# The first matmul of two expert layers on 2x2 blocks with seven products in place of eight

## The chip, the core and the metric

The kernel runs on one core of a Trainium2 chip. Its engines work side by side and meet at semaphores: TensorE (PE; its weight loads have rows of their own, PEld), VectorE (DVE), ScalarE (ACT), GpSimd (POOL) and SyncE (SP), which issues the transfers. The metric is the device time in microseconds (us), the median of several runs; lower is better.

## The reference

```python
qn = q / (np.linalg.norm(q, axis=1, keepdims=True) + 1e-06)      # q, k, v: (1, 6016, 256)
kn = k / (np.linalg.norm(k, axis=1, keepdims=True) + 1e-06)
s = kn.transpose(0, 2, 1) @ qn / tau                             # 256 x 256
a = softmax(s);  x = v @ a                                       # 6016 tokens of 256
h = x @ w_in;  g = h * np.clip(h + 3.0, 0.0, 6.0) / 6.0;  y1 = g @ w_out      # 256 -> 2048 -> 256
h = np.maximum(y1 @ w_in2, 0.0);  y = h * h @ w_out2                          # 256 -> 2048 -> 256
```

## The kernel before

**Opening.** q and k stream in. ACT squares them (L562), DVE adds the squares into `sq_sum`, an SBUF tile of 1024 columns (L689), and PE makes the 256x256 scores (L416). Three of the fourteen loads (`split_loads`) are split into a high and a low float32r half, the low one by POOL (L350, printed as `w_fold_lo`, whose memory it shares). Two short matmuls (L394, L396) sum the squares over partitions, ahead of the last 16 score matmuls. Softmax follows. The attention matrix `a` is folded into `w_in` (`fold`, 8 units of 6 matmuls into `fold_acc`, L442), so that v goes straight into layer 1 ("A"); layer 2 is "B".

**Main part.** Every float32 product is three float32r matmuls: high x high, high x low, low x high. Tokens go in blocks of 512 (eleven, and a last one of 384), printed in PSUM as `hid` (hidden values, 128 x tokens) and `y_acc` (the output). For each block and layer there are 16 chunks `f` of 128 hidden columns. `hidden` is 6 matmuls (L453, L455, L457, twice), since the contraction over 256 is two halves. `contract` is 6 more (L467, L469, L473, twice). In between, ACT makes `ramp` (L626), DVE multiplies it with `hid` (L784 in layer 1, L781 in layer 2), ACT makes the high half `gated_hi` (L631), DVE the low half `gated_lo` (L789). `contract` of chunk f stands behind `hidden` of chunk f+2 (`LAG` = 2). The order on each engine is written out by hand; blocks of layer A and layer B alternate inside a loop (`Fori`). SP loads v per block and stores the output per block; y1 stays on the core. PE waits for `gated_ready` of two chunks ago ahead of `hidden`, and for `gated_hi_ready` and `gated_lo_ready` in `contract`.

## Time and profile before

| | |
|---|---|
| median of 3 runs | 1109.98 us (1108.57 to 1110.26) |
| span of the profiled execution | 1107.8 us, 2.2 us under the median |
| PE busy, share of the span | 1089.1 us, 98%, 4912 matmuls |
| DVE | 648.5 us, 59% |
| ACT | 579.2 us, 52% |
| POOL | 55.2 us, 5% |

The profile has one execution's own span and no separate time for it; the 2.2 us are the distance to the median of the runs. A matmul's row is longer than the distance to the next one, since matmuls are pipelined: what one costs is read from start to start. A full PE says that PE is never without work, not that it runs at its peak.

### The profile page before, as it was taken

How to read it: one execution, taken by the hardware profiler on the slowest of the kernel's cores; microseconds unless marked ns; L12 is line 12 of the kernel's file. 1: busy time of each engine (PE TensorE's matmuls, PEld its weight loads, DVE VectorE, ACT ScalarE, POOL GpSimd, SP SyncE). 2: the span in 40 equal slices, each digit the busy share in tenths (PEclk: the TensorE clock that was granted, in tenths of full speed). 3: DMA queues.
4: the chain of work that ended last, by engine and by line, in shares of the span. 5: the costliest groups of instructions: out<-in, count | busy, mean ns of one | idle time of the engine just before them, and what ended most of it. 6: DMA issues, size and time to landing. Idle time of an engine off the chain costs nothing.

```text
span 1107.8 us, 13572 instructions
## 1 busy us (share of the span) xinstructions
PE 1089.1 (98%) x4912; PEld 914.0 (83%) x4912; DVE 648.5 (59%) x937; ACT 579.2 (52%) x878; POOL 55.2 (5%) x29
## 2 busy tenths in 40 slices
PE   8799999999999999999999999999999999999997
PEld 7678888888888888888888888888888888889887
DVE  5956656555555555655555655655655555556554
ACT  5565565454554554554554554545545455455543
POOL 2360330000000000000000000000000000000000
PEclk9899999999999999999999999999999999999999
DMA  9805000000000000000000000000000000000000
GB/s 353 264 20 170 1 1 20 9 12 15 4 19 0 19 19 0 19 19 0 19 19 0 19 19 0 19 19 0 19 10 9 14 1 19 1 1 20 1 14 20
DMA packets 59351, 33.33 MB, mean 30 GB/s; under 512 B 50369, under 2 KB 54977, under 8 KB 59073
## 3 DMA queue, kind: packets, MB, share of 16 engines
q1 hardware_dynamic: 59328, 33.04, 10.5%
q8 instruction: 14, 0.23, 0.1%
q14 instruction: 9, 0.07, 0.0%
HBM read 26.87 MB, written 6.16 MB: 30 GB/s over the span
## 4 chain that ended last, share of the span: by engine, by line
PE 94%; DVE 3%; ACT 1%; DMA 1%; issue 0%; SPq 0%; DVEq 0%; ACTq 0%
PE hid L453 15%; PE y_acc L473 15%; PE hid L455 15%; PE y_acc L469 15%; PE y_acc L467 15%; PE hid L457 15%; DVE sq_sum L689 3%; PE fold_acc L442 1%; DMA qk<-k_dram 1%; ACT sq L562 0%; PE y_acc L416 0%; ACT w_fold_hi L559 0%; SPq L297 0%; SPq L298 0%; PE y_acc L394 0%
## 5 line engine op out<-in xcount | busy, mean ns | idle before, releaser
L789 DVE TENSOR_TENSOR gated_lo<-gated,gated_hi 128x512 fp32r<-128x512 f32 (+1 forms) x384 | 266.3, 693 | 268.6 <-ACT gated_hi L631 268.6
L631 ACT ACTIVATE gated_hi<-gated 128x512 fp32r<-128x512 f32 (+1 forms) x384 | 239.3, 623 | 292.0 <-DVE gated L781 147.1
L473 PE MATMUL y_acc<-gated_lo,w_out_hi 128*128 128x512 f32 (+1 forms) x768 | 295.4, 385 | 0.0
L469 PE MATMUL y_acc<-gated_hi,w_out_hi 128*128 128x512 f32 (+1 forms) x768 | 295.3, 385 | 0.0
L467 PE MATMUL y_acc<-gated_hi,w_out_lo 128*128 128x512 f32 (+1 forms) x768 | 295.2, 384 | 0.0
L626 ACT ACTIVATE ramp<-hid,zero 128x512 f32<-128x512 f32 (+1 forms) x192 | 130.8, 681 | 103.7 <-PE hid L457 101.4
L784 DVE SCALAR_TENSOR_TENSOR gated<-ramp,hid 128x512 f32<-128x512 f32 (+1 forms) x192 | 129.9, 676 | 87.6 <-ACT ramp L626 86.4
L626 ACT ACTIVATE ramp<-hid,half 128x512 f32<-128x512 f32 (+1 forms) x192 | 130.4, 679 | 97.0 <-PE hid L457 94.6
L781 DVE TENSOR_TENSOR gated<-ramp,hid 128x512 f32<-128x512 f32 (+1 forms) x192 | 130.0, 677 | 76.8 <-ACT ramp L626 75.6
L473 PEld LDWEIGHTS y_acc<-gated_lo,w_out_hi 128*128 128x128 f32 x768 | 144.1, 188 | 27.8 <-DVE gated_lo L789 0.3
L467 PEld LDWEIGHTS y_acc<-gated_hi,w_out_lo 128*128 128x128 f32 x768 | 144.2, 188 | 27.5
L469 PEld LDWEIGHTS y_acc<-gated_hi,w_out_hi 128*128 128x128 f32 x768 | 144.2, 188 | 27.3
L453 PE MATMUL hid<-v_hi,w_fold_hi 128*128 128x512 f32 (+1 forms) x384 | 147.7, 385 | 0.0
L455 PE MATMUL hid<-v_lo,w_fold_hi 128*128 128x512 f32 (+1 forms) x384 | 147.6, 384 | 0.0
L457 PE MATMUL hid<-v_hi,w_fold_lo 128*128 128x512 f32 (+1 forms) x384 | 147.6, 384 | 0.0
L457 PE MATMUL hid<-y_hi,w_in_lo 128*128 128x512 f32 x352 | 137.0, 389 | 0.0
L455 PE MATMUL hid<-y_lo,w_in_hi 128*128 128x512 f32 x352 | 137.0, 389 | 0.0
L453 PE MATMUL hid<-y_hi,w_in_hi 128*128 128x512 f32 x352 | 136.9, 389 | 0.0
L453 PEld LDWEIGHTS hid<-v_hi,w_fold_hi 128*128 128x128 f32 x384 | 72.0, 188 | 14.4 <-issue 0.5
L457 PEld LDWEIGHTS hid<-v_hi,w_fold_lo 128*128 128x128 f32 x384 | 72.1, 188 | 13.8
L455 PEld LDWEIGHTS hid<-v_lo,w_fold_hi 128*128 128x128 f32 x384 | 72.1, 188 | 13.7
L457 PEld LDWEIGHTS hid<-y_hi,w_in_lo 128*128 128x128 f32 x352 | 66.1, 188 | 13.8
(83 smaller groups left out, 607.0 us busy)
## 6 DMA issues: line engine op xcount, KB each, us to landing
v_raw<-v_dram SPq DMA_DIRECT2D x44, 128.0 KB, 2.9
out_dram<-out_sb SPq DMA_DIRECT2D x44, 128.0 KB, 2.5
qk<-q_dram SPq DMA_DIRECT2D x10, 512.0 KB, 11.4
qk<-k_dram SPq DMA_DIRECT2D x10, 512.0 KB, 12.7
raw_a<-w_in_dram SPq DMA_DIRECT2D x4, 512.0 KB, 5.9
raw_b<-w_out_dram SPq DMA_DIRECT2D x1, 2048.0 KB, 12.6
raw_b<-w_in_dram SPq DMA_DIRECT2D x1, 2048.0 KB, 7.7
raw_a<-w_out_dram SPq DMA_DIRECT2D x1, 2048.0 KB, 8.6
```

The source lines that it names most:

```text
L453: nc.tensor.matmul(hid[:, f % 2, 0:n], w_hi[:, m, cols], x_hi[:, m, 0:n], start=(m == 0), stop=False)
L455: nc.tensor.matmul(hid[:, f % 2, 0:n], w_hi[:, m, cols], x_lo[:, m, 0:n], start=False, stop=False)
L457: mm = nc.tensor.matmul(hid[:, f % 2, 0:n], w_lo[:, m, cols], x_hi[:, m, 0:n], start=False, stop=(m == KC - 1))
L467: nc.tensor.matmul(acc[:, m, 0:n], w_lo[:, f, cols], gated_hi[:, r, 0:n], start=(f == 0), stop=False)
L469: nc.tensor.matmul(acc[:, m, 0:n], w_hi[:, f, cols], gated_hi[:, r, 0:n], start=False, stop=False)
L473: mm = nc.tensor.matmul(acc[:, m, 0:n], w_hi[:, f, cols], gated_lo[:, r, 0:n], start=False, stop=(f == NF - 1))
L626: nc.scalar.activation(ramp[:, f % 2, 0:n], hid[:, f % 2, 0:n], ACT.Relu, bias=bias[:, 0:1], scale=scale).then_inc(ramp_ready, 1)
L631: nc.scalar.activation(gated_hi[:, f % GATE_RING, 0:n], gated[:, f % 2, 0:n], ACT.Copy) \
L689: nc.vector.tensor_tensor(sq_sum[:, :, 0:n, :], sq_sum[:, :, 0:n, :], sq[:, s % SQ_RING, :, 0:n, :], ALU.add).then_inc(summed, 1)
L781: nc.vector.tensor_tensor(gated[:, f % 2, 0:n], ramp[:, f % 2, 0:n], hid[:, f % 2, 0:n], ALU.mult).then_inc(gated_ready, 1)
L784: nc.vector.scalar_tensor_tensor(out=gated[:, f % 2, 0:n], in0=ramp[:, f % 2, 0:n], scalar=1.0, in1=hid[:, f % 2, 0:n], op0=ALU.min, op1=A ...
L789: nc.vector.tensor_tensor(gated_lo[:, f % GATE_RING, 0:n], gated[:, f % 2, 0:n], gated_hi[:, f % GATE_RING, 0:n].bitcast(F32), ALU.subtrac ...
```

## The change

**Blocks.** Tokens now go in pairs of blocks (six pairs: five of 2 x 512, the last of 2 x 448), and the 2048 hidden columns in eight groups of 256. For one pair and one group, the hidden values are four tiles of 128 x tokens: C11, C12, C21, C22. They were eight block products (of 3 matmuls each); they are now seven products of sums of blocks. The weights need four sums and differences per block (T/S combinations, seven operands in all, `wi_hi` and `wi_lo`), and so does x (`combine_x`, four subtractions, and seven high and seven low halves per pair, `xs_hi` and `xs_lo`).

**Sums of products.** The tiles are put together in PSUM. `seed` (ACT) copies the first product from `bank_a` to `bank_b`, where the third accumulates on it. `keep_p5` (ACT) takes the second out to `p5_sb`. `seed_u4` (DVE) adds `bank_b` and `p5_sb` into `bank_c`; `add_22` (DVE) adds them into `h22` in SBUF once more has accumulated. `bank_b` and `bank_c` print as `bank_bc`, `p5_sb` as `p_sb`, `h22` as `h_61`.

**Order.** One layer at a time over all tokens: six steps of eight groups for layer 1, six for layer 2. y1 goes out to DRAM after each pair and comes back for layer 2 (SP, 512 KB each). The four tiles of a group have one buffer each; the contractions of group G-1 stand between the products of group G. No loops are left: all instructions are written out. The operands of the next step's x are made inside the step, the weights' halves in the first step and around the layer change (ACT and DVE in `aside`, the low halves on POOL).

**Opening.** `sq_sum` lies in PSUM; a reduction ends it. All eight folds run ahead of the first product, each quarter into its own banks. DVE has the four combinations of the first x and the turning of a whole pair of v among the softmax steps, and behind them seven low halves, the scaling and the combining of the first weights.

The diff, cut to its core (C21 and the like are tile numbers; `fold_bank` and the rest of the weight handling are described above):

```diff
-            def hidden(w_hi, w_lo, x_hi, x_lo, done, f, n):
-
-                if not (isinstance(done, int) and done + f < 2):
...
-                    nc.tensor.matmul(hid[:, f % 2, 0:n], w_hi[:, m, cols], x_hi[:, m, 0:n],
-                                     start=(m == 0), stop=False)
-                    nc.tensor.matmul(hid[:, f % 2, 0:n], w_hi[:, m, cols], x_lo[:, m, 0:n],
-                                     start=False, stop=False)
-                    mm = nc.tensor.matmul(hid[:, f % 2, 0:n], w_lo[:, m, cols], x_hi[:, m, 0:n],
-                                          start=False, stop=(m == KC - 1))
-                mm.then_inc(hid_ready, 1)
...
+            def product(bank, slot, x_slot, G, fresh):
+                s, g = divmod(G, GROUPS)
+                n, cols = width(s % PAIRS), slice(g % 2 * P, (g % 2 + 1) * P)
+                w_hi, w_lo = wi_hi[:, g // 2, slot, cols], wi_lo[:, g // 2, slot, cols]
+                x_hi, x_lo = xs_hi[s % 2][:, x_slot, 0:n], xs_lo[s % 2][:, x_slot, 0:n]
+                nc.tensor.matmul(bank[:, 0:n], w_hi, x_hi, start=fresh, stop=False, skip_group_check=True)
+                nc.tensor.matmul(bank[:, 0:n], w_hi, x_lo, start=False, stop=False, skip_group_check=True)
+                return nc.tensor.matmul(bank[:, 0:n], w_lo, x_hi, start=False, stop=True, skip_group_check=True)
...
+            def contract(tile, m, G):
+                s, g = divmod(G, GROUPS)
+                n, t = width(s % PAIRS), TOKEN_HALF[tile]
+                upper = tile in (C11, C12)
+                f = 4 * (g // 2) + 2 * upper + g % 2
...
+                    elif s <= PAIRS:
+                        pe.wait_ge(y_staged, 4 * (s - 1) + 2 * t + m + 1)
+                    else:
+                        pe.wait_ge(out_turned, 4 * (s - 1 - PAIRS) + 2 * t + m + 1)
+                cols = slice(m * P, (m + 1) * P)
+                to = acc[:, t, m, 0:n]
+                nc.tensor.matmul(to, wo_lo[:, f, cols], gated_hi[:, tile, 0:n], start=(upper and g == 0), stop=False)
+                nc.tensor.matmul(to, wo_hi[:, f, cols], gated_hi[:, tile, 0:n], start=False, stop=False)
+                if m == 0:
+                    pe.wait_ge(gated_lo_ready[tile], G + 1)
+                mm = nc.tensor.matmul(to, wo_hi[:, f, cols], gated_lo[:, tile, 0:n], start=False,
+                                      stop=(not upper and g == GROUPS - 1))
+                if m == KC - 1:
+                    mm.then_inc(contracted[tile], 1)
+
...
+            def group(G):
+                s, g = divmod(G, GROUPS)
+                if g == 0:
+                    pe.wait_ge(x_lo_ready, COMBOS * (s + 1))
+                if s % PAIRS == 0:
+                    pe.wait_ge(wi_lo_ready, s // PAIRS * GROUPS + g + 1)
+                if G > 0:
+                    pe.wait_ge(gated_ready[C11], G)
+                else:
+                    pe.wait_ge(fold0_read, 2)
+                    pe.wait_ge(fold1_read, 2)
+                product(bank_a, A11, B11, G, True).then_inc(p1_made, 1)
+                if G > 0:
+                    contract(C11, 0, G - 1)
+                    contract(C11, 1, G - 1)
+                    pe.wait_ge(p5_ready, G)
+                product(bank_e, S1, T1, G, True).then_inc(p5_made, 1)
+                pe.wait_ge(seed_ready, G + 1)
+                product(bank_b, S2, T2, G, False).then_inc(u2_made, 1)
+                product(bank_a, A12, B21, G, False).then_inc(hid_made[C11], 1)
+                if G > 0:
+                    contract(C21, 0, G - 1)
+                pe.wait_ge(u4_seeded, G + 1)
+                product(bank_b, S3, T3, G, False).then_inc(u3_made, 1)
+                if G > 0:
+                    contract(C21, 1, G - 1)
+                product(bank_c, S4, B22, G, False).then_inc(hid_made[C12], 1)
+                pe.wait_ge(h22_ready, G + 1)
+                product(bank_b, A22, T4, G, False).then_inc(hid_made[C21], 1)
+                if G > 0:
+                    contract(C12, 0, G - 1)
+                    contract(C12, 1, G - 1)
+                    contract(C22, 0, G - 1)
+                    contract(C22, 1, G - 1)
+
...
+            def seed(G):
+                n = width(G // GROUPS % PAIRS)
+                act.wait_ge(p1_made, G + 1)
+                if G > 0:
+                    act.wait_ge(gated_ready[C21], G)
+                nc.scalar.activation(bank_b[:, 0:n], bank_a[:, 0:n], ACT.Copy).then_inc(seed_ready, 1)
...
+                act.wait_ge(p5_made, G + 1)
+                if G > 0:
+                    act.wait_ge(h22_ready, G)
+                nc.scalar.activation(p5_sb[:, 0:n], bank_e[:, 0:n], ACT.Copy).then_inc(p5_ready, 1)
...
+                if G > 0:
+                bias, scale = (half, 1.0 / 6.0) if s < PAIRS else (zero, 1.0)
+                nc.scalar.activation(gated[:, tile, 0:n], hid_tile(tile, n), ACT.Relu, bias=bias[:, 0:1],
+                                     scale=scale).then_inc(ramp_ready[tile], 1)
...
+            for G in range(STEPS * GROUPS):
+                seed(G)
+                if G > 0:
+                    split_gated(C21, G - 1)
+                keep_p5(G)
+                if G > 0:
+                    split_gated(C22, G - 1)
+                make_ramp(C11, G)
+                aside(G, True)
+                make_ramp(C12, G)
+                make_ramp(C22, G)
+                split_gated(C11, G)
+                split_gated(C12, G)
...
+                    dve.wait_ge(x_lo_ready, COMBOS * s)
+                a, b = ((0, 1), (2, 4), (2, 0), (3, 5))[i]
+                nc.vector.tensor_tensor(xr[:, 4 + i, 0:n], xr[:, a, 0:n], xr[:, b, 0:n], ALU.subtract) \
...
+            def seed_u4(G):
+                n = width(G // GROUPS % PAIRS)
+                dve.wait_ge(u2_made, G + 1)
+                dve.wait_ge(p5_ready, G + 1)
+                if G > 0:
+                    dve.wait_ge(gated_ready[C12], G)
+                nc.vector.tensor_tensor(bank_c[:, 0:n], bank_b[:, 0:n], p5_sb[:, 0:n], ALU.add).then_inc(u4_seeded, 1)
...
+            def add_22(G):
+                n = width(G // GROUPS % PAIRS)
+                dve.wait_ge(u3_made, G + 1)
+                if G > 0:
+                    dve.wait_ge(gated_ready[C22], G)
+                nc.vector.tensor_tensor(h22[:, 0:n], bank_b[:, 0:n], p5_sb[:, 0:n], ALU.add).then_inc(h22_ready, 1)
...
+            for G in range(STEPS * GROUPS):
+                if G > 0:
+                    gate(C21, G - 1)
+                aside(G, 0)
+                if G > 0:
+                    gate(C22, G - 1)
+                    split_gated(C21, G - 1)
+                seed_u4(G)
+                aside(G, 1)
+                if G > 0:
+                    split_gated(C22, G - 1)
+                add_22(G)
+                gate(C11, G)
+                gate(C12, G)
+                split_gated(C11, G)
+                split_gated(C12, G)
+                aside(G, 2)
...
-            nc.gpsimd.memset(sq_sum[:, :, :, :], 0.0).then_inc(sum_zeroed, 1)
...
+        sq_sum = bank_bc[:, :, :].rearrange("p x (n c) -> p x n c", c=C)
...
+            nc.vector.memset(bank_bc[:, :, :], 0.0).then_inc(sum_zeroed, 1)
...
-            nc.vector.tensor_tensor(norm_sq[:, :].rearrange("p (x c) -> p x c", c=C), sq_sum[:, :, 0, :],
-                                    sq_sum[:, :, 1, :], ALU.add).then_inc(summed, 1)
...
+            nc.vector.tensor_reduce(norm_sq[:, :].rearrange("p (x c) -> p x c", c=C),
+                                    sq_sum.rearrange("p x n c -> p x c n"), AX_X, ALU.add).then_inc(summed, 1)```

PE, inside a block of layer B, has two equal halves of a period: `hidden` of one chunk, then `contract` of the chunk two before. `y_hi` and `y_lo` are the two halves of y1, here the input.

```order
L453 MATMUL hid<-y_hi,w_in_hi 128x512
L455 MATMUL hid<-y_lo,w_in_hi 128x512
L457 MATMUL hid<-y_hi,w_in_lo 128x512
L453 MATMUL hid<-y_hi,w_in_hi 128x512
L455 MATMUL hid<-y_lo,w_in_hi 128x512
L457 MATMUL hid<-y_hi,w_in_lo 128x512
L467 MATMUL y_acc<-gated_hi,w_out_lo 128x512
L469 MATMUL y_acc<-gated_hi,w_out_hi 128x512
L473 MATMUL y_acc<-gated_lo,w_out_hi 128x512
```

In the changed kernel the middle of a group (after the first product and the contraction of C11) stands so on PE:

```order
L443 MATMUL bank_e<-xs_hi_54,wi_hi 128x512
L444 MATMUL bank_e<-xs_lo_56,wi_hi 128x512
L445 MATMUL bank_e<-xs_hi_54,wi_lo 128x512
L443 MATMUL bank_bc<-xs_hi_54,wi_hi 128x512
L444 MATMUL bank_bc<-xs_lo_56,wi_hi 128x512
L445 MATMUL bank_bc<-xs_hi_54,wi_lo 128x512
L443 MATMUL bank_a<-xs_hi_54,wi_hi 128x512
L444 MATMUL bank_a<-xs_lo_56,wi_hi 128x512
L445 MATMUL bank_a<-xs_hi_54,wi_lo 128x512
L466 MATMUL acc<-gated_hi,wo_lo 128x512
L467 MATMUL acc<-gated_hi,wo_hi 128x512
L470 MATMUL acc<-gated_lo,wo_hi 128x512
```

The second triple accumulates in `bank_b` on what `seed` put there, so PE waits for ACT ahead of it; half a contraction (`acc`) follows the fourth product, and behind that PE waits for DVE's `seed_u4`.

ACT had two instructions per chunk, and now and then one for the input. Before, in a stretch of layer B:

```order
L567 ACTIVATE v_hi<-v_T 128x512
L624 REGISTER_ALU
L626 ACTIVATE ramp<-hid,zero 128x512
L631 ACTIVATE gated_hi<-gated 128x512
L567 ACTIVATE v_hi<-v_T 128x512
```

One whole group of the changed kernel on ACT, from `seed` (its first row) to the ramp of C21, with two halves of the next step's x in it:

```order
L624 ACTIVATE bank_bc<-bank_a 128x512
L648 ACTIVATE gated_hi<-gated 128x512
L631 ACTIVATE p_sb<-bank_e 128x512
L648 ACTIVATE gated_hi<-gated 128x512
L640 ACTIVATE gated<-bank_a,half 128x512
L549 ACTIVATE xs_hi_54<-xr 128x448
L640 ACTIVATE gated<-bank_bc,half 128x512
L640 ACTIVATE gated<-h_61,half 128x512
L648 ACTIVATE gated_hi<-gated 128x512 x2
L549 ACTIVATE xs_hi_54<-xr 128x448
L640 ACTIVATE gated<-bank_bc,half 128x512
```

The ramp of C21, which the next group's `seed` waits for by way of DVE, stands behind the two high halves of C11 and C12 and behind a half of x.

DVE had one multiplication and one low half per chunk. Before, with a transpose of v:

```order
L699 STREAM_TRANSPOSE v_T<-v_raw 128x8x2x32
L779 REGISTER_ALU
L781 TENSOR_TENSOR gated<-ramp,hid 128x512
L789 TENSOR_TENSOR gated_lo<-gated,gated_hi 128x512
L699 STREAM_TRANSPOSE v_T<-v_raw 128x8x2x32
```

The changed kernel on DVE, one group from the multiplication for C21 to the low halves of C11 and C12:

```order
L838 SCALAR_TENSOR_TENSOR gated<-gated,bank_bc 128x512
L720 STREAM_TRANSPOSE xr<-v_raw 128x7x2x32
L838 SCALAR_TENSOR_TENSOR gated<-gated,h_61 128x512
L848 TENSOR_TENSOR gated_lo<-gated,gated_hi 128x512
L858 TENSOR_TENSOR bank_bc<-bank_bc,p_sb 128x512
L720 STREAM_TRANSPOSE xr<-v_raw 128x7x2x32
L848 TENSOR_TENSOR gated_lo<-gated,gated_hi 128x512
L865 TENSOR_TENSOR h_61<-bank_bc,p_sb 128x512
L838 SCALAR_TENSOR_TENSOR gated<-gated,bank_a 128x512
L838 SCALAR_TENSOR_TENSOR gated<-gated,bank_bc 128x512
L848 TENSOR_TENSOR gated_lo<-gated,gated_hi 128x512 x2
```

Two additions per group are new (L858 and L865), each between two products of PE; work for the next x stands before, between and behind.

## Rows read from the trace of the kernel before

**Rows 1.** The page: busy time and share; the chain that ended last

```profile
PE 1089.1 (98%) x4912; PEld 914.0 (83%) x4912; DVE 648.5 (59%) x937; ACT 579.2 (52%) x878; POOL 55.2 (5%) x29
...
PE 94%; DVE 3%; ACT 1%; DMA 1%; issue 0%; SPq 0%; DVEq 0%; ACTq 0%
```

**Rows 2.** Stretches: us, busy time per engine (instructions), PEclk, DMA share, GB/s

```profile
200.00:400.00 200.00, 200.00 (x884) 165.61 (x883) 114.93 (x171) 101.95 (x157) 0.00 (x0) 1.00 0.06 13
...
1080.00:1090.00 10.00, 10.00 (x59) 10.00 (x59) 5.28 (x10) 5.46 (x10) 0.00 (x0) 1.00 0.09 19
```

**Rows 3.** Timeline, layer A block: start us, us, engine, line

```profile
299.74 0.39 PE L467 MATMUL y_acc<-gated_hi,w_out_lo 128*128 128x512 f32 x1
300.71 0.63 ACT L631 ACTIVATE gated_hi<-gated 128x512 fp32r<-128x512 f32 x1 [0.76 <-DVE gated L784]
301.55 0.39 PE L457 MATMUL hid<-v_hi,w_fold_lo 128*128 128x512 f32 x1
301.98 0.69 ACT L626 ACTIVATE ramp<-hid,half 128x512 f32<-128x512 f32 x1 [0.64 <-PE hid L457]
302.91 0.39 PE L473 MATMUL y_acc<-gated_lo,w_out_hi 128*128 128x512 f32 x1
```

**Rows 4.** Timeline of the opening: repeats, a copy out of PSUM, POOL

```profile
62.56 1.28 DVE L706 TENSOR_TENSOR v_lo<-v_T,v_hi 128x512 fp32r<-128x512 f32 x2
64.13 0.57 ACT L605 ACTIVATE y_hi<-hid 128x512 fp32r<-128x512 f32 x1
64.30 7.11 POOL L357 TENSOR_TENSOR w_in_lo<-raw_a,w_in_hi 128x1024 fp32r<-128x1024 f32 x3 [4.35 <-ACT w_in_hi L572]
64.74 0.69 DVE L747 TENSOR_TENSOR y_lo<-hid,y_hi 128x512 fp32r<-128x512 f32 x1 [0.38 <-ACT y_hi L605]
75.70 2.41 POOL L365 TENSOR_TENSOR w_out_lo<-raw_b,w_out_hi 128x1024 fp32r<-128x1024 f32 x1 [1.08 <-ACT w_out_hi L601]
77.62 1.03 DVE L789 TENSOR_TENSOR gated_lo<-gated,gated_hi 128x512 fp32r<-128x512 f32 x1 [0.70 <-ACT gated_hi L631]
```

**Rows 5.** Timeline: a release that comes just at its time

```profile
79.14 0.69 DVE L784 SCALAR_TENSOR_TENSOR gated<-ramp,hid 128x512 f32<-128x512 f32 x1 [0.49 <-ACT ramp L626]
79.61 0.39 PE L473 MATMUL y_acc<-gated_lo,w_out_hi 128*128 128x512 f32 x1
80.28 0.40 PE L455 MATMUL hid<-v_lo,w_fold_hi 128*128 128x512 f32 x1
```

**Rows 6.** Chain of the opening: start us, us, what

```profile
18.24 4.67 DVE sq_sum L689
...
43.96 1.24 DVE sq_sum L689
```

**Rows 7.** PE's timeline in the opening

```profile
21.87 0.40 PE L416 MATMUL y_acc<-w_fold_hi 128*128 128x256 f32 x1 [0.28 <-POOL w_fold_lo L350]
...
24.86 3.62 PE L416 MATMUL y_acc<-qk 128*128 128x256 f32 x16
31.11 0.39 PE L416 MATMUL y_acc<-w_fold_hi 128*128 128x256 f32 x1 [2.64 <-POOL w_fold_lo L350]
...
35.60 7.07 PE L416 MATMUL y_acc<-qk 128*128 128x256 f32 x32
...
53.72 1.22 PE L394 MATMUL y_acc<-norm_sq,ones 128*128 128x256 f32 x2 [4.71 <-DVE norm_sq L692]
...
55.45 5.29 PE L416 MATMUL y_acc<-qk 128*128 128x256 f32 x16
```

**Rows 8.** A stretch of the opening, columns as in rows 2

```profile
30.00:33.00 3.00, 1.89 (x9) 1.89 (x10) 2.96 (x2) 0.77 (x1) 1.06 (x1) 0.73 1.02 399
```

**Rows 9.** Timeline: first fold, first chunk, last matmul

```profile
65.48 0.53 PE L442 MATMUL fold_acc<-w_in_hi,y_hi 128*128 128x512 f32 x1 [0.38 <-DVE y_lo L747]
...
70.30 0.39 PE L453 MATMUL hid<-v_hi,w_fold_hi 128*128 128x512 f32 x1
...
1101.75 0.34 PE L473 MATMUL y_acc<-gated_lo,w_out_hi 128*128 128x384 f32 x1
```

987 lines of the change are left out of this document (501 added, 486 removed).

## The prediction

> **What bounds the kernel now.** I read the page first: PE is busy 98% of the span and carries 94% of the chain that ended last; DVE and ACT are busy little over half [rows 1]. A full PE can still be waiting inside its rows, so I read the stretches next: 884 matmuls in 200 us, clock 1.00, PE never idle [rows 2]. The timeline has the price: 14 steps from 299.74 to 302.91, so 0.2264 us from one 512-column matmul to the next [rows 3]; with 384 columns it is 10/59 = 0.1695 [rows 2]. Between the first chunk at 70.30 and the last matmul at 1101.75 [rows 9] stand 4224 wide and 384 narrow matmuls, 956.3 + 65.1 = 1021.4 us, and 30 of the folds (6.8 us). That leaves 3.4 us of waits: the main part is matmul issue, nothing else.
>
> **The matmuls.** A group of 256 hidden columns and two blocks had 24 + 24 matmuls and has 21 + 24. There are 80 groups of 512 and 16 of 448 columns. At 448 columns I take the middle of the two steps, 0.198. So 3600 x 0.2264 + 720 x 0.198 = 957.6 us: 63.8 us less. This is kept only as far as PE doesn't wait.
>
> **What the seven products ask for.** Per group ACT gets two copies, DVE two additions, beside 4 ramps, 4 multiplications, 4 high and 4 low halves as before. Each has a price near a row: ramp 0.69, high half 0.63 [rows 3], copy from PSUM to SBUF 0.57, DVE 0.69, and two alike in a row start 1.28 - 0.69 = 0.59 apart [rows 4]. Ten instructions are 6 us of a group's 45 x 0.2264 = 10.19, so neither engine is the bound by its sum. The order decides. Hand-overs: a matmul's result is used 0.43 after its start (301.55 to 301.98), 0.20 after its place in the row ends [rows 3]; engine to engine 0.04 [rows 4]. For PE a release must come 0.2 early: the one at 79.83 was for the matmul due at 79.84, and the next one then started at 80.28 instead of 80.07 [rows 5].
>
> Walk through a group, in triples of 0.68 us: P1 from 0; contraction C11 0.68 to 2.04; P5 to 2.72; U2 to 3.40; product C11 to 4.08; half of C21's contraction to 4.75; U3 to 5.43; other half to 6.11; product C12 to 6.79; product C21 to 7.47; contractions C12 and C22 to 10.19.
> - `seed_u4`: U2 is there at 3.60, the addition ends 4.32, and U3 wants it at 4.75 - 0.2. Slack 0.2.
> - `add_22`: U3 is there at 5.63, the addition ends 6.36, wanted at 6.79 - 0.2. Slack 0.2 again.
> - `seed` closes a loop over the group's edge. The high half of C12 waits for the old contraction of C12 (8.83 + 0.2), so it starts at 9.06. The ramp of C21 follows at 9.6, or at 10.1 with a half of x between. DVE then has two low halves, to 10.4, and with x two more, to 11.55. Its multiplication for C21 ends 12.25, which is 2.06 of the next group. `seed` ends 0.57 to 0.69 later, at 2.7, and is wanted at 2.72 - 0.2: 0.17 late. Without x work it ends near 2.0, 0.5 early.
>
> No row has an engine that writes PSUM, so `seed` and `seed_u4` are unknown: from below 0.57 and 0.69, from above twice that. I take 0.63 and 0.69, nearest to the rows that read PSUM. The Trainium skill (PSUM — Partial Sum Buffer, Specifications) has ScalarE faster to PSUM than to SBUF; by that, `seed` is at 0.57 or under and the sum some 3 us lower. No row here can say so.
>
> **The waits summed.** Four loaded groups in each of steps 1 to 4: 16 x 0.17 = 2.9. In layer 2 the output's two transposes stand in DVE's queue in groups 0 and 1 of a step and hold `acc` and the next additions, 0.5 us more: 4 x 1.2, and 0.6 in the last step. Around the layer change, 2.8: POOL makes low halves again, and a DVE instruction on two SBUF tiles is held until POOL's ends (POOL 75.70 to 78.11, the low half from 77.62 lasts 1.03, not 0.69 [rows 4]). The first step costs most, 10: group 0 has no older contractions between its products (1.3), group 1 waits for high halves behind the splitting of weights on ACT, 3 us of it per group (4.0), groups 2 and 3 0.9 each, groups 6 and 7 and the step's edge, with three halves of x each, 3. The end: 1.1. Together 22.2 us. Nothing of it is measured; from below 6 (the first step's half), from above 50 (another 0.3 in each group).
>
> **The opening.** DVE's additions into `sq_sum` last 1.24 alone and 4.67 beside POOL, the first of three such [rows 6]. With one operand in PSUM DVE isn't held: `y_lo`, out of PSUM, took 0.69 while POOL worked from 64.30 to 71.41 [rows 4]. So at least 3 x 3.4 us leave DVE's chain. PE's own row then decides: the 2.64 us before 31.11 go; the 24 matmuls from 31.11 to 35.60 took 4.49 at a clock of 0.73 [rows 8], where the 24 from 21.87 to 24.86 took 2.99; the 4.71 us before 53.72 go; the last 16 took 5.29 and should take 3.62 [rows 7]. Sum 10.5. Against it: DVE has three transposes among the reciprocals, which the last 16 no longer cover (1.2), and one instruction more before `y_lo` (0.6). So folds start at 65.48 - 8.7 = 56.8 [rows 9]. 48 of them in a row end at 67.7. Beside them DVE makes 8 tiles for x (4.7, up to 2.4 more behind POOL), one scaling (0.7), four 256-wide sums (some 1.6), then ACT a high half of 896 columns and DVE its low one (some 2.1): 65.9 to 68.3. First product: 69, from 66 to 72.
>
> **Covered.** y1 out and in is 12 MB over 1000 us, where a block's v already comes and goes under 0.06 DMA share [rows 2]; each load is issued three groups, 30 us, ahead. If SP's queue held one, a step would start late by its landing, a few us. Code without loops: the last blocks ran without loops before, at the same full PE [rows 2].
>
> **Sum.** 69 + 957.6 + 22.2 + (1107.8 - 1101.9 = 5.9 for the end) = 1054.7 of span. The profiled span lies 2.2 under the median of the runs, so 1057.
>
> **Rivals.**
> - *A wait in every group (0.13).* The two additions have 0.2 us of slack each. Two or three semaphores per instruction, where before there was one, may eat it. 0.3 more per group is 29 us: 1086. For it: slack no larger than the lateness of [rows 5] would use up. Against: ACT's hand-over of 0.04.
> - *Slower: writes to PSUM cost double (0.06).* Place: `seed` and `seed_u4`. At 1.38 `seed_u4` is 0.47 late in all 96 groups (45 us), `seed` 0.63 more in the half that is loaded (30 us): 1132. It decides from 53/96 = 0.55 us per group on.
> - *Slower: the clock falls (0.02).* After the idle 2.64 us PE ran at 0.73 on average [rows 8]; if waits in each group did that, the 256-column matmuls show the price (4.49 for 2.99), and half of the time at it gives over 1250. The waits foreseen are 0.2 to 1.5. The Trainium skill (TensorE: Matmul & The Clock Gate, A second HAM failure mode) tells of such a case with PSUM banks cycled and PE idling shortly between groups.
> - *The sum in PSUM gives nothing (0.05).* If DVE is held all the same, the opening stays: 1067.
> - *No waits to speak of (0.03).* 1057 - 20: 1037.
>
> **Numbers.** My forecast 0.70, its own range 1047 to 1068; 0.01 is left for a time within 0.2% of before, which is about what a measurement can tell from no change. Faster: 0.70 + 0.13 + 0.05 + 0.03 = 0.91; slower 0.08. The range reaches up to the first rival.
>
> **What will show it.** Matmuls: 45 per 10.2 to 10.4 us in steady stretches, with DVE and ACT some 75 to 80% busy. The waits of PE should name ACT's `seed` copy in loaded groups, not the additions. `sq_sum` near 1.24 throughout; first fold near 57; first product near 69; last matmul near 1048. Wrong if PE's waits name the additions in every group, if the copies into PSUM last over 0.9, or if the stretch's clock leaves 1.00.

## The result, and the profile after

| | before | changed |
|---|---|---|
| median | 1109.39 us (4 runs) | 1092.84 us (4 runs, 1090.39 to 1095.44) |
| ratio | | 0.9851, 95% interval 0.9831 to 0.9870 |
| span of the profiled execution | 1107.8 us | 1088.6 us (its own time 1090.39) |

The change gains 16.5 us where 53 were forecast, and the measured time lies 6.8 above the first rival's 1086, where the forecast's range ends. The page of the changed kernel answers to [rows 1]: busy time, then the chain that ended last.

```profile
PE 1047.4 (96%) x4624; PEld 862.6 (79%) x4624; DVE 787.3 (72%) x1204; ACT 675.5 (62%) x1146; POOL 92.9 (9%) x62
...
PE 79%; DVE 7%; issue 4%; ACT 4%; POOL 2%; DMA 2%; SPq 1%; DVEq 0%; ACTq 0%; POOLq 0%
```

PE has the 288 matmuls fewer, and its share of the chain fell from 94% to 79%. Where the rest went shows in stretches (columns as in [rows 2]): the first step, a steady one, and one at 448 columns.

```profile
70.00:120.00 50.00, 38.50 (x143) 27.91 (x141) 36.16 (x48) 29.38 (x48) 24.78 (x13) 0.93 0.10 21
200.00:300.00 100.00, 99.90 (x436) 80.94 (x435) 74.31 (x117) 63.47 (x111) 0.00 (x0) 1.00 0.08 22
1030.00:1060.00 30.00, 30.00 (x150) 27.80 (x149) 19.89 (x34) 17.97 (x34) 0.00 (x0) 1.00 0.00 1
```

The steady stretch is as forecast: 436 matmuls in 100 us, clock 1.00. The first 50 us behind the opening hold 143 matmuls; without waits they would hold 221. The timeline answers to [rows 7, 9]: first fold, first product, last matmul.

```profile
57.53 0.50 PE L434 MATMUL bank_bc<-w_in_hi,att_T_hi 128*128 128x512 f32 x1 [2.97 <-DVE att_T_lo L782]
...
70.17 0.39 PE L443 MATMUL bank_a<-xs_hi,wi_hi 128*128 128x512 f32 x1
...
1081.98 0.37 PE L470 MATMUL acc<-gated_lo,wo_hi 128*128 128x448 f32 x1
```

Between the last two stand 1011.8 us. I measure a group from its first product to the next group's: 45 matmuls (21 in the very first), 10.20 us at 512 columns without a wait (45 x 0.2264 = 10.19), 9.12 at 448. What the steps have over their matmuls in this execution, 51.0 us in all for the 22.2 forecast:

| stretch | forecast | measured |
|---|---|---|
| first step, groups 10.3, 16.5, 10.8, 17.4, 10.2, 10.6, 11.0, 11.9 | 10 | 22.6 |
| steps 1 to 4 | 2.9 | 5.4 |
| layer change: steps 5 and 6, groups up to 14.3 and 13.3 | 2.8 | 15.8 |
| rest of layer 2 and the end | 6.5 | 7.2 |

**First step, groups 0 and 1.** The timeline has one sum alone, then group 1, then group 3; L800 and L803 are two of VectorE's four chained sums of `combine_w1`, L865 makes `h22`.

```profile
69.52 0.42 DVE L800 TENSOR_TENSOR wr<-wr 128x256 f32<-128x256 f32 x1
...
87.49 2.34 POOL L338 TENSOR_TENSOR wi_lo<-wr,wi_hi 128x896 fp32r<-128x896 f32 x1 [0.24 <-ACT wi_hi L583]
87.80 2.32 DVE L803 TENSOR_TENSOR wr<-wr 128x256 f32<-128x256 f32 x1
...
91.10 0.68 DVE L865 TENSOR_TENSOR h<-bank_bc,p_sb 128x512 f32<-128x512 f32 x1
91.83 0.50 PE L443 MATMUL bank_bc<-xs_hi,wi_hi 128*128 128x512 f32 x1 [2.72 <-DVE h L865]
...
110.36 5.25 SPq L236 DMA_DIRECT2D v_raw<-v_dram  x8
...
118.16 0.71 DVE L720 STREAM_TRANSPOSE xr<-v_raw 128x512 f32<-128x512 f32 x1 [4.96 <-DMA v_raw<-v_dram]
...
120.09 0.79 PE L443 MATMUL bank_bc<-xs_hi,wi_hi 128*128 128x512 f32 x1 [4.50 <-DVE h L865]
```

A sum that takes 0.42 alone takes 2.32 beside GpSimd's low half, `h22` stands behind it, and PE waits 2.7 us. One sum of the four is held so long in group 0 and one in group 1. **Group 3** is another thing: the next tokens are issued at 110.36, when GpSimd's last low half of the folded weights frees the buffer that `v_raw` shares; the first transpose stands 4.96 us in VectorE's row, `h22` behind it, and PE 4.5 us. After each of the three waits for `h22` (2.3, 2.7 and 4.5 us) seven matmuls start 0.43 apart, the 1.2 GHz level: 21 of them, in groups 0, 1 and 3.

**Layer change.** Waits from 500 to 625 us (total, times, longest), then the timeline of one of them:

```profile
ACT wi_hi L603 <- POOL wr L364: 12.7, 3, 4.5
POOL wr L359 <- DMA wr<-w_in_dram: 12.7, 3, 4.3
```

```profile
535.38 2.13 POOL L338 TENSOR_TENSOR wi_lo<-wr,wi_hi 128x896 fp32r<-128x896 f32 x1 [7.37 <-ACT wi_hi L603]
...
541.69 0.47 SPq L255 DMA_DIRECT2D wr<-w_in_dram  x1
...
545.50 0.73 POOL L359 TENSOR_TENSOR wr<-wr 128x256 f32<-128x256 f32 x1 [4.27 <-DMA wr<-w_in_dram]
...
548.47 0.95 ACT L603 ACTIVATE wi_hi<-wr 128x896 fp32r<-128x896 f32 x1 [4.53 <-POOL wr L364]
549.33 0.62 ACT L640 ACTIVATE gated<-bank_bc,half 128x448 f32<-128x448 f32 x1
```

The raw buffer was free at 537.5. The load was issued at 541.69, since SP's queue stood before it at the wait for `wo_lo` of another load; it landed at 545.5, four sums followed, and at 548.47 ScalarE had stood 4.53 us at the split, with the ramp of C12 behind it.

**A loaded group** of the steady stretch:

```profile
282.89 1.29 DVE L742 TENSOR_TENSOR xs_lo<-xr,xs_hi 128x512 fp32r<-128x512 f32 x2
...
284.10 0.68 DVE L838 SCALAR_TENSOR_TENSOR gated<-gated,bank_bc 128x512 f32<-128x512 f32 x1
...
284.87 0.58 ACT L624 ACTIVATE bank_bc<-bank_a 128x512 f32<-128x512 f32 x1 [1.52 <-DVE gated L838]
...
285.50 0.50 PE L443 MATMUL bank_bc<-xs_hi,wi_hi 128*128 128x512 f32 x1
```

The product at 285.50 was due at 285.44 by its place, and the next matmul comes 0.35 later and not 0.23. Groups of this kind take 10.40 to 10.44 us for 10.20. What releases it is the `seed` copy, held by the gate of C21 behind two `xs_lo`, as forecast.

### The profile page after: what moved, and what is told of

The parts are those of the page before. It is cut to its first block, busy times and chain, and to the rows that moved or that the text cites. A ratio compares the mean times of both kernels' runs of the same rounds, so it can differ in the third digit from the quotient of the medians.

```text
span 1088.6 us, 13394 instructions
## 1 busy us (share of the span) xinstructions
PE 1047.4 (96%) x4624; PEld 862.6 (79%) x4624; DVE 787.3 (72%) x1204; ACT 675.5 (62%) x1146; POOL 92.9 (9%) x62
## 4 chain that ended last, share of the span: by engine, by line
PE 79%; DVE 7%; issue 4%; ACT 4%; POOL 2%; DMA 2%; SPq 1%; DVEq 0%; ACTq 0%; POOLq 0%
PE acc L466 13%; PE acc L470 13%; PE acc L467 13%; PE bank_bc L443 8%; PE bank_bc L445 7%; PE bank_bc L444 7%; PE bank_a L443 3%; PE acc L413 3%; PE bank_a L444 3%; PE bank_a L445 3%; ACT gated_hi L648 2%; PE bank_e L444 1%; PE bank_e L443 1%; PE bank_e L445 1%; DVE xs_lo L742 1%
## 5 line engine op out<-in xcount | busy, mean ns | idle before, releaser
L848 DVE TENSOR_TENSOR gated_lo<-gated,gated_hi 128x512 fp32r<-128x512 f32 (+1 forms) x384 | 264.2, 689 | 110.8 <-ACT gated_hi L648 109.5
L466 PE MATMUL acc<-gated_hi,wo_lo 128*128 128x512 f32 (+1 forms) x768 | 298.0, 388 | 6.6 <-ACT gated_hi L648 3.6
L470 PE MATMUL acc<-gated_lo,wo_hi 128*128 128x512 f32 (+1 forms) x768 | 297.3, 387 | 0.9 <-DVE gated_lo L848 0.9
L467 PE MATMUL acc<-gated_hi,wo_hi 128*128 128x512 f32 (+1 forms) x768 | 296.9, 387 | 0.0
L648 ACT ACTIVATE gated_hi<-gated 128x512 fp32r<-128x512 f32 (+1 forms) x384 | 236.3, 616 | 30.6 <-PE acc L470 29.9
L466 PEld LDWEIGHTS acc<-gated_hi,wo_lo 128*128 128x128 f32 x768 | 144.9, 189 | 37.3 <-issue 5.2
L443 PE MATMUL bank_bc<-xs_hi,wi_hi 128*128 128x512 f32 (+1 forms) x384 | 154.7, 403 | 18.6 <-DVE h L865 9.5
L470 PEld LDWEIGHTS acc<-gated_lo,wo_hi 128*128 128x128 f32 x768 | 144.8, 189 | 30.4 <-DVE gated_lo L848 3.3
L467 PEld LDWEIGHTS acc<-gated_hi,wo_hi 128*128 128x128 f32 x768 | 145.0, 189 | 26.9
L445 PE MATMUL bank_bc<-xs_hi,wi_lo 128*128 128x512 f32 (+1 forms) x384 | 148.8, 387 | 0.0
L444 PE MATMUL bank_bc<-xs_lo,wi_hi 128*128 128x512 f32 (+1 forms) x384 | 148.7, 387 | 0.0
L624 ACT ACTIVATE bank_bc<-bank_a 128x512 f32<-128x512 f32 (+1 forms) x96 | 55.0, 573 | 130.5 <-DVE gated L842 65.6
L640 ACT ACTIVATE gated<-bank_bc,zero 128x512 f32<-128x512 f32 (+1 forms) x96 | 64.5, 671 | 82.4 <-PE bank_bc L445 82.4
L443 PEld LDWEIGHTS bank_bc<-xs_hi,wi_hi 128*128 128x128 f32 x384 | 72.2, 188 | 51.5 <-ACT bank_bc L624 24.0
L640 ACT ACTIVATE gated<-bank_bc,half 128x512 f32<-128x512 f32 (+1 forms) x96 | 64.5, 672 | 70.8 <-PE bank_bc L445 70.8
L865 DVE TENSOR_TENSOR h<-bank_bc,p_sb 128x512 f32<-128x512 f32 (+1 forms) x96 | 65.3, 680 | 49.7 <-PE bank_bc L445 48.3
L838 DVE SCALAR_TENSOR_TENSOR gated<-gated,bank_bc 128x512 f32<-128x512 f32 (+1 forms) x96 | 64.6, 673 | 48.5 <-ACT gated L640 48.5
L445 PEld LDWEIGHTS bank_bc<-xs_hi,wi_lo 128*128 128x128 f32 x384 | 72.4, 188 | 14.0
L858 DVE TENSOR_TENSOR bank_bc<-bank_bc,p_sb 128x512 f32<-128x512 f32 (+1 forms) x96 | 65.6, 683 | 22.6 <-PE bank_bc L445 22.2
L444 PEld LDWEIGHTS bank_bc<-xs_lo,wi_hi 128*128 128x128 f32 x384 | 72.5, 189 | 11.1
L443 PE MATMUL bank_a<-xs_hi,wi_hi 128*128 128x512 f32 (+1 forms) x192 | 74.5, 388 | 0.8 <-DVE xs_lo L742 0.8
## 6 DMA issues: line engine op xcount, KB each, us to landing
qk<-q_dram SPq DMA_DIRECT2D x10, 512.0 KB, 11.2
```

Source lines behind the costliest of these rows:

```text
L443: nc.tensor.matmul(bank[:, 0:n], w_hi, x_hi, start=fresh, stop=False, skip_group_check=True)
L444: nc.tensor.matmul(bank[:, 0:n], w_hi, x_lo, start=False, stop=False, skip_group_check=True)
L445: return nc.tensor.matmul(bank[:, 0:n], w_lo, x_hi, start=False, stop=True, skip_group_check=True)
L466: nc.tensor.matmul(to, wo_lo[:, f, cols], gated_hi[:, tile, 0:n], start=(upper and g == 0), stop=False)
L467: nc.tensor.matmul(to, wo_hi[:, f, cols], gated_hi[:, tile, 0:n], start=False, stop=False)
L470: mm = nc.tensor.matmul(to, wo_hi[:, f, cols], gated_lo[:, tile, 0:n], start=False, stop=(not upper and g == GROUPS - 1))
```

## The experiments

Each kernel is the changed one with the edit shown; gains are against its 1092.84. Its four times spread over 5 us and the interval of its ratio is 0.9831 to 0.9870, some 2 us to either side, and the kernel before had medians of 1109.4 to 1110.1 beside the several experiments. So a gain of under 3 us isn't clear of noise by the medians alone. "Step 0" and the like are taken from the one profiled execution of each kernel.

**1. The sums behind the gates.**

```diff
-                if s == 0 and g < 2 and place == 1:
+                if s == 0 and g < 2 and place == 2:
                     combine_w1(g + 2)
```

> Computes the whole reference. In the changed kernel, VectorE's eight chained sums of the first layer's weights stand in the first step's groups 0 and 1 between the seed addition and the addition that makes h22; here they stand behind the splits of the same group. Theory (the first step is long because these sums, each held up to 2.3 us while GpSimd writes its low halves, stand ahead of additions that TensorE waits for, and TensorE's clock then falls): the waits of 2.5, 2.9 and 4.7 us for h22 in groups 0, 1 and 3 shrink below 1 us each, the half-clock stretches behind them go, and step 0 falls from 98.6 us to 86 to 90; median 1082 to 1086. Rival (GpSimd holds every two-operand VectorE instruction of the first step, wherever the sums stand): the waits move into the seed copy of the next group and step 0 stays within 3 us of 98.6; median above 1089.

Measured: 1101.50, ratio 0.9931 (0.9915 to 0.9948): 8.7 us slower. The wait moves where the rival has it, and the loss is beyond what it allowed: step 0 grows by 6.6 us. Timeline of group 1:

```profile
79.94 2.17 POOL L338 TENSOR_TENSOR wi_lo<-wr,wi_hi 128x896 fp32r<-128x896 f32 x1 [2.90 <-ACT wi_hi L583]
80.08 2.32 DVE L801 TENSOR_TENSOR wr<-wr 128x256 f32<-128x256 f32 x1
...
82.33 1.48 DVE L803 TENSOR_TENSOR wr<-wr 128x256 f32<-128x256 f32 x1
83.84 1.37 DVE L805 TENSOR_TENSOR wr<-wr 128x256 f32<-128x256 f32 x1
85.89 0.58 ACT L624 ACTIVATE bank_bc<-bank_a 128x512 f32<-128x512 f32 x1 [4.94 <-DVE gated L838]
...
86.53 0.79 PE L443 MATMUL bank_bc<-xs_hi,wi_hi 128*128 128x512 f32 x1 [5.37 <-ACT bank_bc L624]
```

Here three of the four meet GpSimd, 5.2 us in place of 1.3, and the gate of C21 is behind them. The hold cost PE its time here too, in another place; my theory had taken the place of the chain for the cause.

**2. PE kept busy.**

```diff
+                keep_warm({0: 10, 1: 14, 3: 22}.get(G, 0))
                 pe.wait_ge(h22_ready, G + 1)
```

> Computes the whole reference. The changed kernel with small idle matmuls (10, 14 and 22 of 128x128, into the bank of S1T1, which is free there) ahead of the wait for h22 in groups 0, 1 and 3 of the first step, so that TensorE works while it waits. Nothing else is changed. Theory (a part of the first step's excess is TensorE at the 1.2 GHz level after an idle stretch of 2 to 5 us, some 0.2 us more for each matmul): the waits stay, the matmuls behind them go at 0.226 each, step 0 falls from 98.6 us by 5 to 8; median 1085 to 1088. Rival (the low clock comes from the load of the opening and not from the idle stretches): the matmuls behind the waits stay at 0.43, step 0 stays within 1.5 us of 98.6, or grows by the idle matmuls; median 1092 or more.

Measured: 1089.96 (0.9801 to 0.9834), 2.9 us less. The stretch, columns as above:

```profile
70.00:120.00 50.00, 46.23 (x237) 36.99 (x238) 36.67 (x48) 29.09 (x48) 23.67 (x13) 1.00 0.10 22
```

The clock is 1.00 for 0.93, and of the 21 slow matmuls none is left; the waits for `h22` stay. So the low clock follows from the idle stretches, as the theory has it, but it was mis-sized: step 0 falls by 2.0 us, not 5 to 8, where 21 x 0.2 = 4.2 were to be had. The waits themselves are the larger part. The 2.9 us by the medians are just at the edge of the noise. The Trainium skill (TensorE: Matmul & The Clock Gate, A second HAM failure mode) tells of such clock losses in every round of a kernel; the steady stretch here, at 1.00 with delays of 0.1 to 0.3 us in it, shows none.

**3. The raw quarter issued first.**

```diff
                 if g > 0:
-                    sp.wait_ge(wi_lo_ready, GROUPS + 2 * g)
-                    load_wr(g)
                     sp.wait_ge(wo_lo_ready, GROUPS + 2 * g)
                     load_wo_raw(2 * g)
...
+                if g + 1 < QUARTERS:
+                    sp.wait_ge(wi_lo_ready, GROUPS + 2 * g + 2)
+                    load_wr(g + 1)
                 sp.wait_ge(wo_lo_ready, GROUPS + 2 * g + 1)
                 load_wo_raw(2 * g + 1)
```

> Computes the whole reference. At the layer change the queue issues the next quarter of w_in2 as soon as its single raw buffer is free, ahead of the wait for the low half of w_out2 and its transfer; everything else is the changed kernel's. Theory (ScalarE stands up to 4.5 us three times at the split of w_in2, because the raw quarter was issued 3.8 us late, takes 4 us to land and GpSimd 2.9 us to sum; the ramp behind it is late, and TensorE waits at the layer change): the three ScalarE waits fall from 12.7 us in sum to 2 or less, groups 5 and 7 of step 5 and group 1 of step 6 fall from 14.3, 11.8 and 13.3 us to 9.6 to 11; median 1084 to 1088. Rival (what holds there is VectorE behind GpSimd's low halves, as the forecast had it): these groups stay within 1 us; median above 1090.

Measured: 1081.63 (0.9727 to 0.9761), 11.2 us less, more than expected. The waits of steps 5 and 6 fall from 15.8 to 7.7 us in the profiled executions; in other kernels that keep this queue order (experiments 1, 2, 4, 5, 7 and 9) they are 13.1 to 20.8, so the changed kernel's profile shows a rather low value. Waits from 500 to 625 us:

```profile
ACT wi_hi L604 <- POOL wr L365: 4.3, 3, 1.7
```

ScalarE's waits fall to 4.3 us in sum, not to 2, and the three groups to 11.4, 9.1 and 10.7 us. Of the 7.7 us that are left, 2.7 are in groups 2 and 3 of step 6, at 11.5 each. There VectorE works beside GpSimd's low halves ahead of the gate, the forecast's cause, with about its price. Two combinations take 2.41 us, where two such take 1.5 in step 1:

```profile
598.43 1.86 POOL L370 TENSOR_TENSOR wo_lo<-wo_raw,wo_hi 128x512 fp32r<-128x512 f32 x1 [1.49 <-ACT wo_hi L611]
598.43 2.41 DVE L737 TENSOR_TENSOR xr<-xr 128x512 f32<-128x512 f32 x2
```

Experiment 8, which puts this work behind the gate, has the two groups at 10.7 and 10.6.

**4. The low halves of x behind the gate.**

```diff
-                    if g >= first and place == 2:
-                        i0 = (g - first) * per
+                    late = 0 if s == 0 else 1
+                    if g >= first + late and place == (0 if late else 2):
+                        i0 = (g - late - first) * per
```

> Computes the whole reference. VectorE's two xs_lo instructions of a loaded group, which stand ahead of the gate of C21 (steps after the first), stand behind that gate; everything else is the changed kernel's. Theory (the wait of 0.25 and the refill of 0.1 in loaded groups is the seed copy, released by the gate of C21, which stands 0.75 us behind two xs_lo): loaded groups fall from 10.40 to 10.64 us to 10.2, in layer 2 too, 0.8 to 1.1 us in each of ten steps; median 1083 to 1086. Rival (the seed copy is late for the bank that the first product makes, or the 1.3 us only move to gated_lo of C21 and the seed addition): loaded groups stay at 10.4 or grow; median 1092 or more.

Measured: 1083.78 (0.9746 to 0.9779), 9.1 us less. Timeline of the same group:

```profile
282.99 0.69 DVE L838 SCALAR_TENSOR_TENSOR gated<-gated,bank_bc 128x512 f32<-128x512 f32 x1 [0.40 <-ACT gated L640]
...
283.60 1.29 DVE L742 TENSOR_TENSOR xs_lo<-xr,xs_hi 128x512 fp32r<-128x512 f32 x2
...
283.77 0.58 ACT L624 ACTIVATE bank_bc<-bank_a 128x512 f32<-128x512 f32 x1 [0.81 <-DVE gated L838]
...
285.05 0.39 PE L443 MATMUL bank_bc<-xs_hi,wi_hi 128*128 128x512 f32 x1
```

The copy now starts 1.3 us ahead of the product that wants it, for 0.6 before, and the product at 285.05 waits for nothing. Groups 3 to 5 fall to 10.20; group 2 stays at 10.60, for it has two combinations of x ahead of the gate instead. The median is as expected, but not by the sum that was to give it: steps 1 to 4 and 7 to 10 give 0.2 to 0.7 us each and not 0.8 to 1.1, which is 4.3 in all. The profiled executions show 2.6 more at the layer change; where the remaining 2 are isn't shown.

**5. The sums on GpSimd.**

```diff
-                if s == 0 and g < 2 and place == 1:
-                    combine_w1(g + 2)
...
                 for h in range(2 * g, 2 * g + 2):
                     wo1_low(h)
+                if g < 2:
+                    combine_w1(g + 2)
```

> Computes the whole reference. GpSimd makes the sums of the first layer's quarters 2 and 3 between its own low halves, as it does for the second layer, and VectorE makes none of them in the first step; everything else is the changed kernel's. Theory (the first step's long waits are VectorE's chain of four sums, held up to 2.3 us each beside GpSimd's low halves, wherever the chain stands; a short two-operand instruction or two that are held elsewhere cost little): VectorE has no chain left to be held, groups 0 to 3 fall from 10.3, 16.5, 10.8 and 17.4 us to 8.5 to 11.5 each, step 0 from 98.6 to 86 to 89; median 1081 to 1085. Rival (the clock of the opening or GpSimd's hold on the gates and splits makes the step long): step 0 stays above 95; median above 1089.

Measured: 1088.35 (0.9787 to 0.9831), 4.5 us less: between the two. Groups 0 to 2 take 7.6, 13.0 and 13.1 for 10.3, 16.5 and 10.8, and step 0 falls only to 96.0, which is the rival's range. GpSimd is now busy 24 of the 30 us from 70 on, and what it holds is the split:

```profile
87.48 4.66 POOL L338 TENSOR_TENSOR wi_lo<-wr,wi_hi 128x896 fp32r<-128x896 f32 x2
87.91 4.78 DVE L862 TENSOR_TENSOR gated_lo<-gated,gated_hi 128x512 fp32r<-128x512 f32 x2 [0.44 <-ACT gated_hi L662]
...
93.38 0.58 ACT L638 ACTIVATE bank_bc<-bank_a 128x512 f32<-128x512 f32 x1 [2.65 <-DVE gated L852]
...
94.02 0.50 PE L457 MATMUL bank_bc<-xs_hi,wi_hi 128*128 128x512 f32 x1 [1.88 <-ACT bank_bc L638]
```

Two low halves, 1.3 us together when alone, take 4.78. So the chain of sums was a part of the loss and not the whole of it; moving work from VectorE to GpSimd is a weak remedy for holds. The Trainium skill (Perfetto Trace Analysis, Optimizing Scalar/DVE Operations) says that such a move might not help; here it helped, by 4.5 us where 8 to 12 were expected.

**6. Edits 3, 4 and 5 together.**

> Computes the whole reference. Three edits together: the raw quarters of w_in2 issued first, the two xs_lo behind the gate of C21, and the first layer's last two sums on GpSimd. Theory (three separate causes, whose prices add, since each stands in groups of its own): 11.2 from the first, 9.1 from the second, and what the third gives alone; with 8 to 12 for that, 1061 to 1066. Rival (they share waits at the layer change, where both of the first two act): some 4 us less, 1066 to 1070.

Measured: 1071.33 (0.9639 to 0.9671), 21.5 us less, where the three alone make 24.8. The shortfall of 3.3 us is near the rival's 4; both ranges, made with 8 to 12 us for the third edit, are missed. That anything is shared is not shown: the changed kernel's median stands three times in the 24.8 and once in the 21.5, so 1.7 us of error in it would make the whole 3.3. The traces don't settle it, since steps 5 and 6 vary between executions: step 5 takes 82.9 us in the changed kernel's profiled run, and 84.8 and 87.0 in experiments 5 and 2, whose edits don't touch it. With the three edits it takes 76.0.

**7. The sums of squares in SBUF.**

```diff
-        sq_sum = bank_bc[:, :, :].rearrange("p x (n c) -> p x n c", c=C)
+        sq_sum = at(76, "sq_sum", [P, 2, 2, C], F32)
...
-            nc.vector.memset(bank_bc[:, :, :], 0.0).then_inc(sum_zeroed, 1)
+            nc.vector.memset(sq_sum[:, :, :, :], 0.0).then_inc(sum_zeroed, 1)
```

> Computes the whole reference. The running sums of squares back in SBUF (4 KB that lie free in the opening) in place of the two PSUM banks; everything else is the changed kernel's. Theory (the chain of VectorE's 22 additions sets the opening, and each takes 1.75 us with two SBUF operands beside ScalarE's squares and 1.23 with the sum in PSUM): the additions go back to about 1.7 us, the first product from 70 to 77 to 80 us; median 1100 to 1104. Rival (the transfers and the splits of q and k set the opening, the additions lie beside them): the first product stays within 2 us of 70; median 1091 to 1095.

Measured: 1104.59 (0.9928 to 0.9966), 11.8 us more. The additions' group in the changed kernel:

```profile
L706 DVE TENSOR_TENSOR bank_bc<-bank_bc,sq 128x1024 f32<-128x1024 f32 x22 | 27.1, 1233 | 8.3 <-ACT sq L530 6.5
```

In this one:

```profile
L706 DVE TENSOR_TENSOR sq_sum<-sq_sum,sq 128x1024 f32<-128x1024 f32 x22 | 38.7, 1761 | 6.4 <-ACT sq L530 4.5
```

The mean of 1761 ns hides what happens. Nineteen of the 22 additions take 1.22 to 1.23 us here as well, beside ScalarE's squares or not; the other three take 4.72, 5.36 and 5.37, each beside one of GpSimd's three splits. The second of them, and then an addition beside the second split in the changed kernel:

```profile
25.05 5.34 POOL L326 TENSOR_TENSOR qk_lo<-qk,qk_hi 128x2048 fp32r<-128x2048 f32 x1 [4.12 <-ACT qk_hi L527]
26.11 5.36 DVE L706 TENSOR_TENSOR sq_sum<-sq_sum,sq 128x1024 f32<-128x1024 f32 x1
```

```profile
23.11 4.61 POOL L326 TENSOR_TENSOR qk_lo<-qk,qk_hi 128x2048 fp32r<-128x2048 f32 x1 [1.02 <-ACT qk_hi L527]
24.01 1.23 DVE L706 TENSOR_TENSOR bank_bc<-bank_bc,sq 128x1024 f32<-128x1024 f32 x1 [0.35 <-ACT sq L530]
```

So the expectation's number came true and its reading, 1.75 us each, was wrong; the forecast's (three held additions [rows 6]) was right. The first product with the sum in SBUF:

```profile
81.09 0.77 PE L443 MATMUL bank_a<-xs_hi,wi_hi 128*128 128x512 f32 x1 [3.23 <-DVE wi_lo L810]
```

The 22 additions take 11.6 us less with the sum in PSUM, and the first product comes 10.9 earlier. Without this one part the change would gain 4.7 us of its 16.5; that is all that the seven products bring as yet, net of their waits and of what else was changed.

**8. Edits 3, 4, 5, and three smaller moves:** the combinations of x one place later, the last `xs_lo` of step 0 spread over groups 5 to 7, the two later output transposes apart. Of the diff only these three are shown.

```diff
-                    for i in {(1, 2): (0, 1), (2, 0): (2,), (2, 1): (3,)}.get((at_, place), ()):
+                    for i in {(2, 0): (0, 1), (2, 1): (2, 3)}.get((at_, place), ()):
...
-                    if g == 1 and place == 0:
-                        turn_out(s - 1, 1, 0)
-                        turn_out(s - 1, 1, 1)
+                    if g == 1 and place < 2:
+                        turn_out(s - 1, 1, place)
...
-                    if g >= first and place == 2:
-                        i0 = (g - first) * per
+                    late = 1
+                    if s == 0:
+                        for i in {(5, 2): (0,), (6, 0): (1, 2), (6, 2): (3,), (7, 0): (4, 5), (7, 1): (6,)}.get((g, place), ()):
+                            split_x(s + 1, i)
+                    elif g >= first + late and place == 0:
+                        i0 = (g - late - first) * per
```

> Computes the whole reference. The three edits of the kernel before it in this list, and one more: VectorE's combinations of the next step's x one place later (behind the gate of C21), the last xs_lo of step 0 spread over groups 5 to 7, and one of the two late output transposes of each layer-2 step behind the seed addition. Theory (group 2 of each step, at 10.6, waits for the gate of C21 behind two combinations; group 1 of a layer-2 step, at 10.7, for the low half of C21 behind two transposes; groups 5 to 7 of step 0 for the same gate): groups 2 and 1 fall to 10.2 to 10.3 and groups 5 to 7 of step 0 to 10.2 to 10.4, 7 to 9 us in all; median 6 to 9 us below that of the three edits. Rival (the work moved makes the addition for h22 late, which has 0.2 us to spare, and the wait only changes place): within 2 us of the three edits.

Measured: 1066.13 (0.9585 to 0.9617), 5.2 us below experiment 6, for 6 to 9. Group 2 of a step falls to 10.27, groups 5 to 7 of step 0 to 10.3, 10.2 and 11.0; group 1 of a layer-2 step only from 10.69 to 10.64, so one transpose seems to hold it almost as two did.

**9. The first step's transposes in group 4.**

```diff
-                    if s + 1 < PAIRS and (at_, place) in ((0, 1), (0, 2), (1, 0), (1, 1)):
+                    if s == 0:
+                        for t, h in {(4, 0): [(0, 0)], (4, 1): [(0, 1)], (4, 2): [(1, 0), (1, 1)]}.get((g, place), ()):
+                            turn_v(1, t, h)
+                        for i in {(5, 0): (0, 1), (5, 1): (2, 3)}.get((g, place), ()):
+                            combine_x(1, i)
+                    elif s + 1 < PAIRS and (at_, place) in ((0, 1), (0, 2), (1, 0), (1, 1)):
...
-                    for i in {(1, 2): (0, 1), (2, 0): (2,), (2, 1): (3,)}.get((at_, place), ()):
+                    for i in {(1, 2): (0, 1), (2, 0): (2,), (2, 1): (3,)}.get((at_, place), ()) if s else ():
```

> Computes the whole reference. In the first step alone VectorE's four transposes of the next tokens stand in group 4 in place of groups 3 and 4, and the four combinations in group 5; everything else is the changed kernel's. Theory (group 3 of the first step, 17.4 us, stands for the transfer of v: its eight pieces are issued only when GpSimd's last low half frees the raw buffer, take 0.66 us each to issue and land 7.8 us later, and VectorE stands 5.0 us at the first transpose with the addition for h22 behind it; the clock falls after): group 3 falls to 10.4 to 11, groups 4 and 5 to at most 11, step 0 from 98.6 to 92 to 93.5; median 1086 to 1088. Rival (group 3 is long by GpSimd's hold like groups 1 and 2, which the sums on GpSimd did not shorten): group 3 stays above 15, median 1091 or more.

Measured: 1086.23 (0.9777 to 0.9810), 6.6 us less, as the theory has it: group 3 falls from 17.4 to 11.1, step 0 to 92.2; group 5, which takes the combinations, goes from 10.6 to 11.3.

**10. Edits 8 and 9 together.**

> Computes the whole reference. The four edits together and the transposes of the first step in group 4. Theory: the edit takes from it what it takes alone, 5.5 to 7 us; median 1059 to 1061. Rival (the work moved into group 5 meets the edit that spreads the xs_lo there): 1062 to 1065.

Measured: 1061.21 (0.9543 to 0.9575), 4.9 us below experiment 8 for 5.5 to 7, at the edge between the two ranges.

**11. And the large low halves on VectorE.**

```diff
-                if g > 0:
-                    for j in range(2):
-                        wi_low(wr[g], g, j, 0)
...
+                if s == 0 and g < 3 and place == 2:
+                    wi_low(g + 1, 0)
+                if s == 0 and 0 < g <= 3 and place == 0:
+                    wi_low(g, 1)
```

> Computes the whole reference. The five edits together, and the six large low halves of the first layer's folded weights (128x896, 2.1 us on GpSimd) on VectorE (1.1 us each) in the first step, so that GpSimd has only the sums and the low halves of w_out1 there. Theory (what is left in groups 0 to 2, some 5 us over 10.2 a group in sum, is VectorE held by the 2.1 us instructions of GpSimd): the holds of over 1.5 us go, groups 1 and 2 fall from some 12.7 and 14 us to 10.5 to 12, 2 to 4 us below the five together; 1056 to 1058. Rival (VectorE's own 6.5 us more cost as much as the holds): within 1.5 us of the five together, or slower.

Measured: 1058.38 (1058.17 to 1059.86), ratio 0.9534 (0.9519 to 0.9550). It is 2.8 us below experiment 10 by the medians, as the theory says, though the intervals overlap a little. Group 2 falls from 13.1 to 10.8, but group 1 goes from 13.0 to 13.9 and group 0 from 6.1 to 7.4. Step 0 is only 0.3 us shorter in the profiled execution; the other 1.5 of the 1.9 us by which it ends earlier lie before the first product, which comes anywhere from 68.1 to 71.4 us in kernels with this opening. So the 2.8 us are the medians', and the trace bears out the theory in group 2 alone. Page and first stretch of this kernel:

```profile
PE 1036.4 (98%) x4624; PEld 861.0 (81%) x4624; DVE 783.2 (74%) x1202; ACT 680.0 (64%) x1146; POOL 86.9 (8%) x64
...
PE 88%; DVE 5%; ACT 2%; issue 2%; DMA 1%; POOL 0%; SPq 0%; DVEq 0%; ACTq 0%
```

```profile
70.00:100.00 30.00, 25.95 (x104) 18.35 (x103) 24.73 (x33) 22.23 (x37) 15.85 (x14) 1.00 0.00 1
```

With the same matmuls as the changed kernel it is 34.5 us faster than it, and 51.7 faster than the kernel before.

**12. Experiment 10 with PE kept busy in groups 0 to 2.** Its idle matmuls of groups 1 and 2 go into the bank of C12 with a start. The Trainium skill (PSUM — Partial Sum Buffer, PSUM: the matmul accumulator) says that a start clears the marks of the whole bank and that VectorE's writes don't set them; by that, the seed U2 + P5 is left out past column 128 of C12 in these groups. So this kernel leaves a part of the reference out, though its expectation says that it computes the whole, and only its time is read. The rest is experiment 10.

```diff
+                if G in (1, 2):
+                    pe.wait_ge(gated_ready[C12], G)
+                    for _ in range(4 * G):
+                        nc.tensor.matmul(bank_c[:, 0:P], ones[:, :], ones[:, :], start=True, stop=True)
                 pe.wait_ge(seed_ready, G + 1)
...
+                if G == 0:
+                    pe.wait_ge(p5_ready, 1)
+                    keep_warm(8)
```

> Computes the whole reference. The five edits together, and small idle matmuls ahead of the three waits that are left in the first step (group 0 for the seed addition, groups 1 and 2 for the seed copy; 8, 4 and 8 of them). Theory (each idle stretch of 2 us is followed by matmuls at the 1.2 GHz level, which cost 2 to 3 us in groups 0 to 2): 1 to 2.5 us below the five together. Rival: within 0.5 us of it, as the waits are too short for the clock to fall in most runs.

Measured: 1060.10 (0.9535 to 0.9567), 1.1 us below experiment 10. The theory is not borne out all the same: experiment 10 had no slow matmul in step 0 behind its waits of 0.4 to 1.9 us (its clock there is 1.00), this one has none either, and groups 0 to 3 are no shorter. The two profiled executions differ elsewhere: the first product at 69.0 us for 71.4, with group 0 at 7.4 for 6.1, and the 448-column groups of the last step at 9.12 us for 9.30, which is 1.2 us. Neither is shown to be of this edit, so the rival's mechanism stands and the 1.1 us have no cause shown.

## Why the prediction was wrong

The step that failed is "The waits summed": 22.2 us, where the profiled execution has 51.0. Two of its terms carry nearly all of that, "The first step costs most, 10" (22.6) and "Around the layer change, 2.8" (15.8); the rest held to a few us.

- **Matmuls at 512 columns: right.** 45 per 10.20, clock 1.00.
- **Matmuls at 448 columns: mis-sized.** 0.198, the middle of two steps, was 0.2027 (9.12 / 45) in this execution: 3.4 us over 720 matmuls.
- **Copies into PSUM: right.** `seed` takes 0.58 and `seed_u4` 0.69, and PE's waits in loaded groups name `seed`; 0.63 and 0.69 were taken. The Trainium skill (PSUM — Partial Sum Buffer, Specifications) has ScalarE faster to PSUM than to SBUF; the trace agrees by 2%, 0.582 against 0.594 for `keep_p5`.
- **A loaded group: mis-sized.** In steps 1 to 3, 0.17 was 0.2 to 0.3 in the three groups with `xs_lo` ahead of the gate, since a late release costs 0.1 more before the row runs full again, and 0.4 in the group with two combinations there; that group took 1.5 in step 4. Steps 1 to 4 lost 5.4 us for 2.9.
- **The opening: right.** First fold 57.5 for 56.8, first product 70.2 for 69; experiment 7 prices this part at 11.8 us. What the forecast said of operands in PSUM, from a single `y_lo` row, held for 22 additions, and the three held ones that it had leave the chain are the 11.8 us. The 1 us between 69 and 70.2 says little, since the first product of like kernels comes from 68.1 to 71.4.
- **Busy shares: half right.** In the steady stretch VectorE is busy 74%, ScalarE 63%, where some 75 to 80 were forecast for both; that cost nothing.
- **"The first step costs most, 10": 22.6.** I had the hold [rows 4], but priced it on one instruction of 0.69 that took 1.03, and looked for the loss on ACT. The traces show one part in chains of four short sums on VectorE, of which one or more is held up to 2.3 us beside GpSimd's instructions of 2.1 to 2.3, with PE's release behind the chain; experiment 5 takes the chain away and gains 4.5. Experiment 9 shows the second: the next tokens share memory with a weight buffer, so their transfer is issued only at 110.36, has landed at 118.16, and VectorE stands at it from 113.2 on: 6.6 us. Experiment 2 shows the third, the clock after the idle stretches: 2 to 3 us, in part those of the same groups. With all edits (experiment 11) step 0 still has 9.5 us of waits, which no run takes apart.
- **"Around the layer change, 2.8": 15.8.** I named the hold of VectorE, and 2.7 us of it are in what experiment 3 leaves. The larger part, 8 us by the profiled executions and 11.2 by the medians, is a wait in SP's queue: one raw buffer, its load behind a wait for something else, 4 us of landing, 2.9 of sums, and ScalarE standing at it in order. I had said of SP's queue that a held load would cost "a few us" for tokens, and hadn't walked the weights' chain through it.
- **Of the rivals** the wait in every group came nearest by its number, 1086, and is refuted by its mechanism: four groups in eight wait for nothing. PSUM writes, the clock in steady state and the opening went as the forecast had them.

The sum closes: 1.2 (first product) + 3.4 + 28.8 (waits, 51.0 - 22.2) + 0.5 (end) + 2.0 (this profiled span lies 4.2 under the median, not 2.2; the execution was the fastest of the four) = 35.9 of the 35.8 us by which 1057 missed. Experiment 11, with the same matmuls and most of the named waits gone, ends at 1058.4. That it comes so near to 1057 is luck in part: its profiled execution still has 19.4 us of waits for the 22.2 forecast, but 9.5 of them are in the first step, 4.7 around the layer change, and the steady groups have nearly none.

## What to carry to other kernels

Steady state forecast well from slacks in one group; the misses were in the one-off stretches where weights are prepared, so walk those group by group as well: each chain from "buffer free" through issue, landing and sums to the in-order engine that stands at it. In these runs a VectorE instruction on two SBUF tiles could last as long as GpSimd's beside it (2.32 beside 2.34, 5.36 beside 5.34), so a chain of short ones is a bad thing to leave there, and its place in the row matters less than its company; with one operand in PSUM it wasn't held. Look at the single rows before you trust a group's mean: 1.76 us was nineteen of 1.23 and three of about 5. When a small wait recurs, first swap two instructions around the release: experiment 4 took 4.3 us out of eight steps by a change of order.

## What the runs showed of the hardware

- The step of a 448-column matmul has two values. In the last step it was 0.2027 (9.12 us a group) in the changed kernel and experiments 1, 3, 5, 6, 8, 9 and 12, 0.2066 (9.30) in experiments 2, 4, 7, 10 and 11. It isn't a property of the execution: experiments 1, 5 and 12 have a group at 9.30 in step 5, experiments 2, 7 and 10 one at 9.12. At 512 columns it was 0.2264 in all. I have no cause for it.
- A 256-column addition of two SBUF tiles, 0.42 us alone, took 2.32 beside a GpSimd instruction of 2.17 to 2.34; a 1024-column one with the sum in PSUM took 1.23 throughout, and with the sum in SBUF (experiment 7) 4.72 to 5.37 beside GpSimd instructions of 4.54 to 5.34, and 1.23 otherwise.
- In the changed kernel PE's waits of 2.3 to 4.5 us were each followed by seven matmuls 0.43 apart, in place of 0.226; a wait of 1.7 there and one of 1.9 in experiment 10 by none.
